# Moving the attention-times-V matmuls behind the transposes, and spreading the dense work over more slots

## The reference

```python
# 1. recurrence, per batch and head, over t
y[:, :, t] = einsum('bhd,bhde->bhe', rt, state)
Sa = einsum('bhde,bhe->bhd', state, at)
state = state * wt[:, :, None, :] - einsum('bhd,bhe->bhde', Sa, bt) + einsum('bhd,bhe->bhde', vt, kt)

# 2. four attention experts of 64 channels, the best two of them weighted per position
for e in range(4):
    q, k, v = x @ wq[e], x @ wk[e], x @ wv[e]
    a = softmax(causal(q @ k.T / 8))
    out += weight_if_in_top_2(e) * (a @ v @ wo[e])

# 3. gated MLP that mixes positions
h = relu(x @ w_in); u, v = h[..., :512], h[..., 512:]
v_s = einsum('ts,bsd->btd', w_spatial, normalised(v)) + b_spatial
return (u * v_s) @ w_out
```

## Time and profile before

| what | us |
|---|---|
| median of 3 runs | 1037.37 |
| lowest and highest | 1037.13, 1043.01 |
| the profiled execution, its own time | 1037.13 |
| its span in the profile | 1035.3 |
| TensorE (PE) busy | 970.0 |
| VectorE (DVE) busy | 521.4 |
| ScalarE (ACT) busy | 461.1 |
| GpSimd (POOL) busy | 243.6 |

### The profile page before, as it was taken

The page is one execution under the profiler, slowest core; times in us unless marked ns, Lnnn a source line. Parts: engine busy times, 40 slices in busy tenths (PEclk is TensorE's granted clock), DMA queues, the critical chain, the costliest instruction groups (busy, mean ns, idle before and its releaser), DMA issues.

```text
span 1035.3 us, 36907 instructions
## 1 busy us (share of the span) xinstructions
PE 970.0 (94%) x15696; PEld 706.8 (68%) x15696; DVE 521.4 (50%) x1440; ACT 461.1 (45%) x1122; POOL 243.6 (24%) x350
## 2 busy tenths in 40 slices
PE   2889999999999999999987999999999999999988
PEld 1778888888887888876645655566555665557455
DVE  5567877777777777754334234322433124341220
ACT  5455565555654655643245243442433423434401
POOL 7444535444344344321000000100011000110011
PEclk9999999999999999999999999999999999999989
DMA  3233443444334334251230100001000000000001
GB/s 119 72 91 106 117 133 100 124 141 124 97 96 128 95 96 130 68 135 40 64 135 1 39 1 1 1 26 52 0 1 1 27 13 0 1 1 26 14 0 39
DMA packets 50644, 63.49 MB, mean 61 GB/s; under 512 B 26544, under 2 KB 36592, under 8 KB 50480
## 3 DMA queue, kind: packets, MB, share of 16 engines
q1 hardware_dynamic: 50480, 61.13, 20.0%
HBM read 53.22 MB, written 7.86 MB: 59 GB/s over the span
## 4 chain that ended last, share of the span: by engine, by line
PE 80%; DVE 10%; issue 4%; ACT 3%; DMA 1%; POOL 1%; SPq 0%; DVEq 0%; ACTq 0%
PE banks L1489 13%; PE banks L618 7%; PE banks L1388 6%; PE banks L669 6%; PE banks L1429 5%; PE banks L1441 4%; PE banks L1501 4%; PE banks L1471 4%; PE banks L1458 4%; PE banks L1407 4%; DVE state_z L1052 3%; PE banks L854 3%; PE banks L844 3%; PE banks L1374 3%; PE banks L716 3%
## 5 line engine op out<-in xcount | busy, mean ns | idle before, releaser
L488 ACT ACTIVATE powers_z<-powers,parity 128x256 f32<-128x256 f32 x240 | 108.6, 500 | 172.0 <-DVE powers L920 172.0
L1268 POOL TENSOR_TENSOR v_st<-v_st,u_t 128x384 f32<-128x384 f32 x32 | 31.9, 997 | 497.8 <-DVE v_st L1638 497.8
L1489 PE MATMUL banks<-w_st,v_n 128*128 128x384 f32 x384 | 140.6, 502 | 4.9 <-issue 4.9
L669 PE MATMUL banks<-pq,powers_z 64*64 64x64 f32 (+1 forms) x3072 | 136.2, 228 | 9.2 <-issue 4.6
L669 PEld LDWEIGHTS banks<-pq,powers_z 64*64 64x64 f32 x3072 | 115.1, 141 | 15.8 <-issue 6.5
L450 POOL TENSOR_TENSOR state<-state_sum,dc 128x160 f32<-128x160 f32 x92 | 68.7, 746 | 177.8 <-DVE state_sum L1038 177.8
L1273 ACT ACTIVATE probs_t<-banks 128x512 f32<-128x512 f32 (+1 forms) x96 | 52.0, 542 | 129.8 <-PE banks L1429 129.8
L1489 PEld LDWEIGHTS banks<-w_st,v_n 128*128 128x128 f32 x384 | 69.0, 193 | 52.7 <-issue 16.1
L1030 DVE SCALAR_TENSOR_TENSOR vu_tok<-banks,minus,vz_tok 128x80 f32<-128x80 f32 x192 | 48.9, 296 | 71.2 <-PE banks L854 71.2
L1584 DVE CUSTOM_DVE_ANT_0 probs<-banks,hide 128x128 f32<-128x128 f32 (+5 forms) x96 | 56.0, 621 | 54.5 <-PE banks L1407 54.1
L1287 ACT ACTIVATE probs<-probs,neg_max 128x128 f32<-128x128 f32 (+5 forms) x96 | 63.2, 660 | 35.9 <-DVE neg_max L1584 35.9
(11 more groups left out here) (162 smaller groups left out, 1849.4 us busy)
## 6 DMA issues: line engine op xcount, KB each, us to landing
w_all<-decays_dram SPq DMA_DIRECT2D x48, 160.0 KB
w_all<-kb_ch_dram SPq DMA_DIRECT2D x48, 160.0 KB
vz_tok<-vz_tok_dram SPq DMA_DIRECT2D x24, 320.0 KB, 3.4
r_all<-rz_ch_dram SPq DMA_DIRECT2D x48, 160.0 KB
x_dram<-y_tok SPq DMA_DIRECT2D x384, 10.0 KB, 1.9
a_raw<-a_ch_dram SPq DMA_DIRECT2D x48, 80.0 KB
vc_tok<-vc_tok_dram SPq DMA_DIRECT2D x24, 160.0 KB, 3.7
r_all<-r_ch_dram SPq DMA_DIRECT2D x48, 80.0 KB
```

The costliest lines, as they stand in the source:

```text
L488: act.activation(powers_z[:, i, :, j, :], powers[:, i, :, :], ACT.Copy, scale=parity[:, j:j + 1])\
L669: ins = pe.matmul(to[r, k * n:k * n + n], powers_z[r, i, k, :, :].rearrange("p j t -> p (j t)"), right, start=True, stop=True)
L1489: ins = pe.matmul(bank[M_BANK + j % 2][:, 0:TH], v_n[:, i, d * P:d * P + P], w_st[:, i, t], start=(i == 0), stop=(i == BLOCKS - 1))
```

## The change

The slot list now has pieces + 2 entries in every step: one after `scores`, one after each piece, one after `times_v`, so 61 slots with the one ahead of the steps. On TensorE all pieces of a step, each with a slot behind it, now stand ahead of `times_v`. ScalarE and VectorE walk through the new list in the same sense; ScalarE's order of copies and exponentials stays.

```diff
-        slots = [(-1, 0)] + [(s, k) for s in range(STEPS + 3) for k in range(max(1, len(pieces_of(s))))]
+        slots = [(-1, 0)] + [(s, k) for s in range(STEPS + 3) for k in range(len(pieces_of(s)) + 2)]
...
-                        count = len(pieces_of(s))
-                        for k in range(max(2, count)):
-                            if k < count:
+                        last = len(pieces_of(s)) + 1
+                        for k in range(max(2, last)):
+                            if k + 1 < last:
                                 turned(n, pieces_of(s)[k])
                             if k < 2 and s < STEPS:
                                 exponentials(n, s, k)
-                            if k + 1 < count:
+                            if k + 1 <= last:
                                 outputs(n, dense_from(n, s, k + 1), dense_upto(n, s, k + 1))
...
                         slot(n, s, 0)
+                        for k, piece in enumerate(pieces_of(s)):
+                            turn(n, piece)
+                            slot(n, s, k + 1)
                         if s >= 3:
                             times_v(n, s - 3)
-                        for k, piece in enumerate(pieces_of(s)):
-                            if k > 0:
-                                slot(n, s, k)
-                            turn(n, piece)
+                        slot(n, s, len(pieces_of(s)) + 1)
...
-                        last = max(1, len(pieces_of(s))) - 1
+                        last = len(pieces_of(s)) + 1
                         spatial(n, dense_from(n, s, 0), dense_upto(n, s, last))
```

## The result

Over 20 runs of each kernel the changed one took 1046.38 us in the median (1041.72 to 1050.77), the one before 1038.69 (1031.06 to 1051.98). The ratio is 1.0069 with a 95% interval of 1.0048 to 1.0091: 7 us slower, within 1%. The forecast was 1040.3, 3.2 above the profiled execution before, and its range of 1029 to 1046 is 8 less to 9 more than that execution; the 7 us lie within it. The median of 1046.38 itself lies just over 1046, the kernel before having taken 1.3 us more in these 20 runs than in its first three. The new profiled execution took 1043.48 us with a span of 1041.7.

A forecast was written before the change was run, and what follows sets the result against it. The prediction took the kernel as bound by TensorE, busy 94% of the span, with only its gaps to win. 1037.13 - 7.5 (batch 0) + 10.8 (thin slots) + 0.5 - 0.6 gave 1040.3 us, range 1029 to 1046.

The forecast's parts named there:

- Batch 0, -7.5: Attention of batch 0: with `times_v` behind the transposes, waits of TensorE go, 7.5 us less.
- Thin slots, +10.8: Batches 1 to 3: one dense unit between pieces leaves waits on copies, 3.6 us a batch, 10.8 us more.
- its sign in the profile: Batches 1 to 3: about ten waits a batch of 0.3 to 0.4 us before L1429 on `probs_t` copies.
- First slot, +0.5: Slot ahead of the steps: falls to one unit, so `scores` waits for the last `k_t` copy, 0.16 us a batch.
- Batch ends, -0.6: Each batch's end: the share piece no longer comes last, so three waits of 0.2 us go, 0.6 less.
- Change of form: Batches 1 to 3: turns between `times_v`, `scores`, pieces and dense units, replaced 36 times; taken as 0, 2 us for the range.
- Sum: Whole kernel: 1037.13 - 7.5 + 10.8 + 0.5 - 0.6 = 1040.3 us.
- The first: Batches 1 to 3: short waits don't show and only batch 0 counts, 1029.0 us; chance 0.20.
- the 1.38 us: Least time from the start of a four-block piece to the next piece that needs its bank.
- The second: Batch 0 gains only half, as second copies come late without `times_v` as cover, 1043.8 us; chance 0.15.
- The third: Batches 1 to 3: late exponentials make second pieces of steps 6 to 11 wait 0.9 us more, 1057 us; chance 0.05.
- The fourth, the clock: Batches 1 to 3: short waits bring the half clock level once a batch at 1.3 us, 1044.2 us; chance 0.06.

The follow-up runs named there:

- Experiment one: The kernel before, with `times_v` moved behind the transposes in batch 0 only; ratio 0.9878 (0.980 to 0.9956).
- experiment two: The changed kernel with batch 0 back in the old order, `times_v` ahead of the transposes; 1055.6 us in one run, beside 1044.9 for the kernel before.
- experiment three: The kernel before, its 33 slots kept, with `times_v` behind the transposes in all batches; ratio 0.9832 (0.9771 to 0.9893).
- four: The changed kernel's 61 slots, but `times_v` ahead of the transposes, between two slots; 1063.6 us in one run.
- experiment five: The kernel before with two slots a step, around `times_v`, and no dense unit between the pieces; 1098.0 us in one run.
- experiment seven: The changed kernel once more, unaltered, against the kernel before; ratio 1.0068 (1.0030 to 1.0106).
- nine: The kernel before against itself; ratio 0.9979 (0.9946 to 1.0013).

## Why the prediction was right, point by point

The letters are those of the prediction: P for a piece of transposes, V for `times_v`, S for `scores`, d for a dense unit.

- **Batch 0, -7.5:** measured -8.2. In steps 10 to 12 the waits came as laid out, counted by starts: 0.5 to 0.6 in four places (the last of them laid out as 0.16 and 0.34), 1.2 before the share, and none before `times_v`. Experiment one isolates the term. The low clock did go, worth 1.0 us by experiment two and not 1.3. Most of the 0.7 us that the term was short lies in steps 4 to 9: they fell from 20.8 us (532.97 to 553.78) to 17.45 (534.74 to 552.19), 3.4 and not 2.8. The prediction had about 1.3 us of waits come there before the later pieces; the list has the same two ahead of pieces, 0.56 and 0.34, in both traces.
- **Thin slots, +10.8:** measured 3.6 a batch, 10.7 in all, in the twelve places forecast. Experiments three to five show it by removing the cause, by bringing it back in the old order, and by taking it to its full size. What the prediction had wrong is its sign in the profile: it promised some ten listed waits a batch, and the list has four.
- **First slot, +0.5:** the first unit takes 0.91 to `scores` (617.73 to 618.64) instead of 0.74, 0.17 a batch.
- **Batch ends, -0.6:** -1.2, since the transposes of a new batch ran without the listed 0.21 and without the part that is not listed.
- **Change of form, taken as 0 with 2 us either way:** this is the term that was mis-sized. What is left of 13.6 is 2.4 us. A unit behind `times_v` takes 0.85 to `scores` (660.60 to 661.45), which is 0.2 over its 0.645, 0.1 a side. So V to d costs 0.1, where V to P cost 0.05, and 36 times 0.05 is 1.8 of the 2.4; the prediction kept 0.05 to the good and to the bad and chose the middle, and 2.4 lies a little past its 2.
- **Sum:** +3.2 forecast, +4.2 in the stages, +7 in the timed ratio. That the stages come within 1.0 us of the forecast is in part luck: 2.4 us of change of form left out, against 1.3 too little taken off in batch 0 and at the batch ends. The interval of the ratio starts at 5.0 us (at 3.1 in experiment seven). The recurrence, the same code in all kernels, took between 503.1 and 515.5 us in the eleven traces of this study, and the kernel before was profiled at the lowest of these. In the runs beside the experiments the kernel before had medians of 1042.28 to 1045.01 us, against 1038.69 in the first 20, which points at spread in that first set for a part of the last 3 us. It is not shown: a recurrence that the change lengthens by so much in the mean is not excluded, and the cause stays open.

**Rivals.** The first (short waits don't show) falls with the 1.38 us. The second (half the gain in batch 0) falls with experiment one. The third (exponentials start late) did not appear, not even in experiment five, where every step from a piece of four blocks to the next took 1.37 to 1.41. The fourth, the clock, did not appear in the changed kernel, where the clock stood at 1.00 behind gaps of 0.3 to 0.4 us; in experiment five, behind gaps of 0.75 to 0.97, it fell to 0.50 in one or two places a batch. The rule of the Trainium skill that small idle times between groups of matmuls can make the clock fall again and again (TensorE: Matmul & The Clock Gate, "A second HAM failure mode: psum-queue depth-cycling") was thus not borne out by the trace of the change, and the trace of experiment five agrees with it.

## What to carry to other kernels

A change can mix two edits that work in different places: moving `times_v` won 8 us where no filler existed, and spreading the filler evenly lost 14, of which 11 were waits where the filler had just covered a latency. Before thinning the work between two uses of one PSUM bank, add up the time from the first transpose to the start of the copy, the copy and the release (here 0.64 + 0.60 + 0.14 = 1.38 us), and keep at least that much from the start of one use to the start of the next. Here evenness won nothing. And on a saturated engine count by starts, not by the list of waits, which left out the part of a gap that lay under the row of the matmul before it (0.30 us unlisted, 0.40 listed as 0.24).

## What the runs showed of the hardware that I had not expected

- The same wait of 2.1 us at the same place in batch 0 left the clock at 1.00 in one execution and brought it to about 0.5 in others. Five traces have it: in experiment two the clock stayed and the stage took 47.67 us; in the kernel before, in four, five and nine the clock fell, and it took 48.65, 48.96, 48.96 and 49.04.
- Part of the spread of the whole kernel's time goes with such stretches of the recurrence. In the execution of experiment one, with a recurrence of 515.5 us, the windows (5 us each) show two falls that the trace of the kernel before does not have at these places, where its clock stays at 1.00. Ahead of them TensorE had been idle for part of a window (busy 3.24 and 2.69 of 5.00 us):

```profile
395.00:400.00 5.00, 3.24 (x44) 2.60 (x44) 0.91 (x3) 1.67 (x4) 0.00 (x0) 0.73 0.34 84
400.00:405.00 5.00, 5.00 (x134) 4.58 (x133) 3.17 (x8) 2.09 (x5) 0.76 (x1) 0.50 0.19 45
455.00:460.00 5.00, 2.69 (x82) 2.39 (x81) 1.93 (x5) 0.86 (x3) 0.76 (x1) 0.88 0.51 108
460.00:465.00 5.00, 5.00 (x105) 4.13 (x105) 1.84 (x7) 2.42 (x7) 0.00 (x0) 0.50 0.28 80
```

  The clock is not all of it. The recurrences of experiments three and five had a single fall, as that of the kernel before, and took 507.3 and 507.0 us against 503.1; what else differed no run isolates.

- Going from `times_v` straight to `scores` cost nothing measurable, while either of the two next to a dense unit cost 0.1 us (1.02 us from `times_v` to `scores` in experiment three; 0.85 us for a unit of 0.645 between the two in the changed kernel). Over three batches that order with thick slots won 3.3 us.
